# Sliding-window attention ahead of two expert layers: a dilated head's values loaded by a second queue, plain outputs kept in place, copies and denominators divided between VectorE and ScalarE

## The reference

```python
def _attn_ref(q, k, v):                      # each (4, 8, 576, 64): batch, head, position, width
    window, dilation = 32, 4
    scores = scale * np.matmul(q, k.transpose(0, 1, 3, 2))
    rel = pos[:, None] - pos[None, :]
    mask_plain = (rel >= 0) & (rel < window)
    mask_dil = (rel >= 0) & (rel < window * dilation) & (rel % dilation == 0)
    masks = np.stack([mask_plain if h < H // 2 else mask_dil for h in range(H)], axis=0)
    scores = np.where(masks[None, :, :, :], scores, -1000000000.0)
    scores = scores - np.max(scores, axis=-1, keepdims=True)
    attn = np.exp(scores)
    attn = attn / (np.sum(attn, axis=-1, keepdims=True) + 1e-09)
    return np.matmul(attn, v).astype(np.float32)

x = attn_out.transpose(0, 2, 1, 3).reshape(B * S, H * D)   # 2304 token rows of 512
x = _moe_ref(x, ...)       # each row to the best of 8 experts: relu(x @ w1) @ w2, times a gate
return _moe2_ref(x, ...)   # h = x @ w_in; (h * cos(h)) @ w_out
```

## Time and profile before

| | |
|---|---|
| median of 3 runs | 851.77 us (851.12 to 851.94) |
| the profiled execution: its time | 852.95 us |
| its span, first to last instruction | 851.1 us |
| mean granted TensorE clock | 0.996 |
| busy: PE / PEld / DVE / ACT / POOL | 97% / 89% / 72% / 58% / 9% |
| DMA | 93.79 MB, mean 110 GB/s |

### The profile page before, as it was taken

How to read it: one execution, slowest core, us unless ns; L and a number is a source line. 1 busy time by engine, 2 the same in 40 slices (tenths; PEclk the granted TensorE clock), 3 DMA queues, 4 the chain that set the end, 5 groups by cost and what they waited for, 6 DMA issues and landing times.

```text
span 851.1 us, 15552 instructions
## 1 busy us (share of the span) xinstructions
PE 824.1 (97%) x5046; PEld 755.6 (89%) x5046; DVE 610.3 (72%) x1187; ACT 490.4 (58%) x948; POOL 75.5 (9%) x129
## 2 busy tenths in 40 slices
PE   7999999989999999999999999999999999999994
PEld 6877877789999999999989999989999998999993
DVE  6888887885655655555587777798777788777762
ACT  3557767644554554444466666676666676666652
POOL 3122112150100000000000000011000003000002
PEclk9999999999999999999999999999999999999998
DMA  6497886355535434433431221223121214122001
GB/s 149 96 232 177 193 208 183 82 161 161 185 125 162 149 118 131 149 125 123 149 101 59 66 73 52 75 87 112 51 75 50 75 49 149 59 66 68 8 1 74
DMA packets 114913, 93.79 MB, mean 110 GB/s; under 512 B 65816, under 2 KB 94488, under 8 KB 114848
## 3 DMA queue, kind: packets, MB, share of 16 engines
q1 hardware_dynamic: 109920, 78.81, 32.1%
q0 software_dynamic: 4928, 14.16, 5.1%
HBM read 83.51 MB, written 9.44 MB: 109 GB/s over the span
## 4 chain that ended last, share of the span: by engine, by line
PE 86%; DVE 4%; SPq 3%; issue 3%; ACT 2%; DMA 1%; POOL 0%; DVEq 0%; POOLq 0%; ACTq 0%
PE bank L765 25%; PE bank L763 25%; PE bank L764 25%; PE bank L625 2%; PE bank L604 2%; PE bank L588 1%; SPq L378 1%; PE bank L613 1%; SPq L357 1%; DMA xtok<-x_rows 1%; PE bank L805 1%; DVE shifted L1277 1%; DVE row_max L1274 1%; PE bank L706 1%; ACT probs L947 1%
## 5 line engine op out<-in xcount | busy, mean ns | idle before, releaser
L765 PE MATMUL bank<-yh,up_h 128*128 128x384 f32 x384 | 129.6, 338 | 0.0
L763 PE MATMUL bank<-yh,up_l 128*128 128x384 f32 x384 | 129.6, 337 | 0.0
L764 PE MATMUL bank<-yl,up_h 128*128 128x384 f32 x384 | 129.1, 336 | 0.0
L765 PE MATMUL bank<-dn_h,hid 128*128 128x512 f32 x288 | 114.0, 396 | 0.0
L764 PE MATMUL bank<-dn_l,hid 128*128 128x512 f32 x288 | 113.8, 395 | 0.0
L763 PE MATMUL bank<-dn_h,hid 128*128 128x512 f32 x288 | 112.5, 391 | 0.8 <-DVE hid L1604 0.7
L1142 ACT ACTIVATE work<-bank 128x384 f32<-128x384 f32 x96 | 47.2, 491 | 79.6 <-PE bank L765 78.8
L1350 DVE TENSOR_TENSOR dn_l<-dn_raw,dn_h 128x512 fp32r<-128x512 f32 (+1 forms) x79 | 71.8, 909 | 28.1 <-ACT dn_h L998 27.9
L1086 ACT ACTIVATE hid<-bank 128x352 fp32r<-128x352 f32 x64 | 29.8, 465 | 106.4 <-PE bank L765 104.0
L1154 ACT ACTIVATE work<-work 128x384 f32<-128x384 f32 x96 | 50.5, 526 | 64.0 <-DVE work L1599 64.0
L1594 DVE TENSOR_SCALAR work<-work 128x384 f32<-128x384 f32 x96 | 34.7, 362 | 70.6 <-ACT work L1142 70.2
(11 more groups left out here) (213 smaller groups left out, 1727.7 us busy)
## 6 DMA issues: line engine op xcount, KB each, us to landing
up_raw<-in_moe_w_dram SPq DMA_DIRECT2D x32, 512.0 KB, 4.4
dn_raw<-in_moe_w_dram SPq DMA_DIRECT2D x32, 512.0 KB, 3.6
up_raw<-in_moe_w_in_dram SPq DMA_DIRECT2D x24, 512.0 KB, 3.4
dn_raw<-in_moe_w_out_dram SPq DMA_DIRECT2D x24, 512.0 KB, 3.5
qn<-in_q_dram SPq DMA_DIRECT2D x32, 144.0 KB, 2.8
kn<-in_k_dram SPq DMA_DIRECT2D x32, 144.0 KB, 3.3
xtok<-x_rows SPq DMA_DIRECT2D x4, 1152.0 KB, 7.6
x_rows<-osb POOLq DMA_DIRECT2D x8, 288.0 KB, 3.5
```

Source lines behind the costliest of these rows:

```text
L763: mm(o, w[1], x[0], start=first, stop=False, skip_group_check=True)
L764: mm(o, w[0], x[1], start=False, stop=False, skip_group_check=True)
L765: return mm(o, w[0], x[0], start=False, stop=last, skip_group_check=True)
```

## The change

The line numbers in the diff are left out; names are as above.

- **Values of dilated heads.** SyncE loads those of the pair's first head only (four DMAs). GpSimd loads the second head's into the same buffer (`load_second_head`), behind its store of the plain pair two before, counted by a new semaphore `head1_v_in`, for which TensorE waits beside `v_in`.
- **Outputs of plain heads.** The multiply writes them into `xtok` itself, and GpSimd stores them to `x_rows` from there (`plain_stored`, awaited only ahead of the gather). The read-back brings the right half of the columns only, those of the dilated heads.
- **Keys.** VectorE copies the second half of one head (1) only; ScalarE copies that of head 0, a third instruction behind its two, with a semaphore `k_head` for which a pair's first scores wait as well.
- **Denominators.** ScalarE makes them (Copy with bias 1e-9), in each step ahead of the exponential and, where there are any, behind the query copies. VectorE waits for them ahead of the reciprocal.
- **Expert weights.** In the last batch SyncE waits for the second head's last values before it issues the four weight loads.

```diff
...
-    QK_IN, PLAIN_IN, DIL_IN = 16 * 4, 16 * 2 * 3, 16 * 2 * 4
-    STORES = 16 * 5
+    QK_IN, PLAIN_IN, DIL_IN = 16 * 4, 16 * 2 * 3, 16 * 4
+    STORES = 16 * 4
...
-        osb = [sb2(f"osb{i}", [QT, NT, 2, D]) for i in range(2)]
+        osb = [sb2(f"osb{i}", [QT, NT, 2 * D]) for i in range(2)]
...
-        def half_out(copy, p, half, first=False):
-
-            for h in range(2):
+        def half_out(copy, p, half, first=False, heads=(0, 1), signal=None):
+
+            for h in heads:
...
-            last.then_inc(tr_out[half], 1)
+            last.then_inc(signal or tr_out[half], 1)
...
-                        for t, j0, j1, r, i0 in V_PARTS:
+                        for t, j0, j1, r, i0 in V_PARTS if h < 1 else ():
                             sp.dma_start(vw[slot][j0:j1, t:t + 4:3, h, 0:D], vr[r, i0:i0 + j1 - j0]).then_inc(v_in[slot], 16)
...
-                sp.dma_start(xtok[:, bass.ds(last * NT, NT), :],
-                             x_rows[bass.ds(last * S, S), :].rearrange("(t p) c -> p t c", p=QT)).then_inc(x_in, 16)
+                sp.dma_start(xtok[:, bass.ds(last * NT, NT), DM // 2:],
+                             x_rows[bass.ds(last * S, S), DM // 2:].rearrange("(t p) c -> p t c", p=QT)).then_inc(x_in, 16)
...
                         with sp.If(b > B - 2):
+                            sp.wait_ge(head1_v_in[1], B * DIL_IN)
                             load_expert(0, 0, 0, 2)
...
+            def load_second_head(b, p):
+
+                pool.wait_ge(pv_done, b * STEPS + 3 * p + 3)
+                pool.sem_inc(carrier, 1)
+                vr = v[bass.ds(b, 1), 2 * p + 1].rearrange("o (i a r) d -> r i (o a) d", a=2, r=2)
+                for t, j0, j1, r, i0 in V_PARTS:
+                    pool.dma_start(vw[p % 2][j0:j1, t:t + 4:3, 1, 0:D], vr[r, i0:i0 + j1 - j0]).then_inc(head1_v_in[p % 2], 16)
+
...
-                        pool.dma_start(xb.rearrange("(t p) c -> p t c", p=QT), o).then_inc(stored[slot], 16)
+                        pool.dma_start(xb.rearrange("(t p) c -> p t c", p=QT),
+                                       xtok[:, bass.ds(b * NT, NT), 2 * p * D:2 * (p + 1) * D]).then_inc(plain_stored, 16)
+                        load_second_head(b, p + PAIRS // 2)
...
+            pool.wait_ge(plain_stored, B * PAIRS // 2 * 16)
             pool.wait_ge(ids_ready, 1)
...
                         pe.wait_ge(tr_out[half], b * 2 * PAIRS + 2 * p + 3)
+                    pe.wait_ge(k_head, b * PAIRS + p + 1)
...
+                    if p >= PAIRS // 2:
+                        pe.wait_ge(head1_v_in[p % 2], (b + 1) * DIL_IN)
...
                 half_out(lambda o, x: A(o, x, ACT.Copy), p, 0, first)
+                act.wait_ge(tr_done, b * 4 * PAIRS + 4 * p + 12)
+                half_out(lambda o, x: A(o, x, ACT.Copy), p, 1, first, (0,), k_head)
+
+            def denominators(b, s):
+
+                act.wait_ge(pv_done, b * STEPS + (s + 7))
+                act.wait_ge(inv_done, b * STEPS + (s + 3))
+                s %= STEPS
+                A(denom[:, s % 2, :], bank[6 + s % 2][:QT, 0:4 * VN].rearrange("p (a c) -> p a c", a=4)[:, :, D],
+                  ACT.Copy, bias=1e-9).then_inc(denom_done, 1)
...
                         next_pair(b, s, q_out)
+                    if s >= 2:
+                        denominators(b, s - 2)
+                    else:
+                        before_this(act, b, lambda: denominators(b, s - 2))
                     exps(b, s)
...
-                half_out(cp, p, 1, first)
+                half_out(cp, p, 1, first, (1,))
...
+                if p < PAIRS // 2:
+                    rows = xtok[:, bass.ds(b * NT + 2 * u, 2), 2 * p * D:2 * (p + 1) * D]
+                else:
+                    rows = osb[p % 2][:, 2 * u:2 * u + 2, :]
...
-                dve.wait_ge(pv_done, G(7))
-                ts(denom[:, s % 2, :], o[:, :, D], 1e-9, None, ALU.add).then_inc(denom_done, 1)
                 dve.wait_ge(denom_done, G(3))
                 V.reciprocal(inv[:, s % 2, :], denom[:, s % 2, :]).then_inc(inv_done, 1)
...
```

More of the change, by code:

```diff
@@ L199, in fused_kernel @@
         v_in = [sem(f"v_in{i}") for i in range(2)]
+        head1_v_in = [sem(f"head1_v_in{i}") for i in range(2)]
         tr_done = sem_from("tr_done", 8)
         tr_out = [sem_from(f"tr_out{i}", 1) for i in range(2)]
+        k_head = sem("k_head")
         init_v = sem("init_v")
@@ L210, in fused_kernel @@
         denom_done = sem_from("denom_done", 2)
-        inv_done = sem_from("inv_done", 2)
+        inv_done = sem_from("inv_done", 4)
         norm_done = sem_from("norm_done", 4)
         stored = [sem(f"stored{i}") for i in range(2)]
+        plain_stored = sem("plain_stored")
         x_in = sem("x_in")
@@ L521, in _ @@
                     pool.wait_ge(norm_done, b * STEPS + 3 * p + 7)
-                    o = osb[slot][:].rearrange("p t h c -> p t (h c)")
+                    o = osb[slot]
                     xb = x_rows[bass.ds(b * S, S), 2 * p * D:2 * p * D + 2 * D]
                     if p < PAIRS // 2:
-                        pool.dma_start(xb.rearrange("(t p) c -> p t c", p=QT), o).then_inc(stored[slot], 16)
+                        pool.dma_start(xb.rearrange("(t p) c -> p t c", p=QT),
+                                       xtok[:, bass.ds(b * NT, NT), 2 * p * D:2 * (p + 1) * D]).then_inc(plain_stored, 16)
+                        load_second_head(b, p + PAIRS // 2)
                     else:
@@ L988, in _ @@
             probsT_out(B, -1)
+            denominators(B, -2)
+            denominators(B, -1)
             def weights_hi(w, which, raw, hi, i, J, per, slots_free, parts=1, part=0):
@@ L1286, in normalise @@
                 o = bank[6 + s % 2][:QT, 0:4 * VN].rearrange("p (a c) -> p a c", a=4)
-                if u == 0:
-                    if p >= PAIRS // 2:
-                        dve.wait_ge(stored[p % 2], b * STORES + 16)
-                    else:
+                if p < PAIRS // 2:
+                    rows = xtok[:, bass.ds(b * NT + 2 * u, 2), 2 * p * D:2 * (p + 1) * D]
+                else:
+                    rows = osb[p % 2][:, 2 * u:2 * u + 2, :]
+                    if u == 0:
                         def slot_stored():
@@ L1295, in normalise @@
                         before_this(dve, b, slot_stored)
-                dve.wait_ge(pv_done, G(7))
-                ts(denom[:, s % 2, :], o[:, :, D], 1e-9, None, ALU.add).then_inc(denom_done, 1)
                 dve.wait_ge(denom_done, G(3))
                 V.reciprocal(inv[:, s % 2, :], denom[:, s % 2, :]).then_inc(inv_done, 1)
-                dve.wait_ge(inv_done, G(3))
-                tt(osb[p % 2][:, 2 * u:2 * u + 2, :, :].rearrange("p t h c -> p (t h) c"), o[:, :, 0:D],
-                   inv[:, s % 2, :].unsqueeze(2).broadcast_to([QT, 4, D]), ALU.mult).then_inc(norm_done, 1)
+                dve.wait_ge(inv_done, G(5))
+                tt(rows.rearrange("p t (h c) -> p t h c", h=2), o[:, :, 0:D].rearrange("p (t h) c -> p t h c", t=2),
+                   inv[:, s % 2, :].rearrange("p (t h) -> p t h", t=2).unsqueeze(3).broadcast_to([QT, 2, 2, D]), ALU.mult).then_inc(norm_done, 1)
             def over_e(x):
```

## The result

| | before | after |
|---|---|---|
| median of 11 runs each | 852.5 us (851.12 to 855.02) | 847.46 us (846.04 to 849.97) |
| span of the profiled execution | 851.1 us | 845.6 us |
| time less span, wherever both are on record | 1.83 to 1.97 us | 1.49 to 1.60 us |
| ratio | | 0.9934 (0.9922 to 0.9947) |

The ratio on the 851.77 us of the forecast gives 846.1 us: 5.6 us less (4.5 to 6.6), where 3.2 were forecast. Two later measurements of the changed kernel, on other chips, gave 0.9947 (0.9930 to 0.9963) and 0.9923 (0.9898 to 0.9948).

The account below looks back on a forecast made before the run. One latency chain per pair, from scores to exponential and transpose, held back by VectorE's key copies, was taken to set the pace. Start 1.00 and 13 pairs 2.16 gave 3.16 us off 851.77: 848.6 us, range 847.2 to 851.4.

Parts of the forecast that it names:

- The pair's pace, 7.73: Attention, per pair of heads: 7.73 us in place of 7.83, the row maximum waiting for scores alone, if ScalarE keeps up.
- The walk: ScalarE's queue, step by step through a pair: denominators' waits cost nothing; third key copy ends at 81.98, wanted at 82.09.
- Values on two queues: Dilated heads' value loads: SyncE's saved issues bring nothing; GpSimd's loads stay hidden.
- The read-back: Token rows at batch boundaries: 576 KB in place of 1152 land in 5 us, before first use; 0.86 us come back.
- Rival 2: Read-back still late because pieces, not bytes, set its time: the 0.86 us stay, 849.5 us; chance 0.08.
- GpSimd in time with 2.0 us to spare: GpSimd's four value loads: landed some 5.8 us after the multiply, first used 7.83 us after, so hidden.
- ScalarE's slots: Time added on ScalarE: 0.37 us per third key copy, 0.10 per denominator, hidden in the pair, narrowly behind square sums.
- rival 1: ScalarE's slots as long as durations (denominator 0.32, copy 0.41): 1.85 us lost in five pairs, 850.5 us; chance 0.18.
- Rival 3: A pair's first scores wait for ScalarE's third key copy: 0.4 us more per pair, 853.8 us, slower; chance 0.09.
- The address instruction: VectorE, ahead of the multiply into token rows in half the steps: between nothing and 0.1 us, taken as nothing, covered.
- Expert weights: SyncE, last batch: weight loads wait for values until about 134.6, wanted at 144.15; no cost, up to 1 us if stores compete.
- The start, 1.00: First batch, three places where VectorE alone holds it: 0.12, 0.46 and 0.42 us, together 1.00, bounds 0.5 and 1.4.

Follow-up runs that it names:

- both copies shared: Kernel before with denominators and third key copy on ScalarE, values and outputs as before: ratio 1.0005 (0.9985 to 1.0026).
- the run with the filled gap: Changed kernel with the next pair's query transposes and copies one step earlier, where TensorE waits for the third step's exponential: 848.22 us, 0.9933.
- copies undone: Changed kernel with key copies and denominators back on VectorE, split values and direct rows kept: 850.40 us, 0.9990.
- four small additions: Kernel before plus one each: needless copy, semaphore instruction between waits, third key copy's wait, denominator's wait: 853.73, 853.56, 852.98, 851.65 us.

## Why the prediction was right or wrong, point by point

**The bound and the mechanism: right.** The pace was set by the chain from scores to exponential, and VectorE's second key copy held it up. The row maximum now starts 0.04 us after the scores, and TensorE's gap shrank from 0.63 to 0.52 us: the 0.10 of the forecast. The runs with one part agree: with denominators alone VectorE keeps both key copies, and the pair stays at 7.70, 0.12 more than with the third key copy alone.

**The pair's pace, 7.73: wrong by 0.15, the term that made most of the miss.** The step that failed is "In a pair TensorE's weight loads run without a gap except once". There are two gaps. The walk followed the one of 0.63 us, to the exponential and the transposes, and not the one of 0.15 us behind them (83.96 to 84.11), in which TensorE waits for the copy of the previous step's probabilities that stands behind the exponential on ScalarE (ends at 84.06). It was taken as TensorE's own work, which nothing could shorten. In the changed kernel it is gone: from transposes to product 0.38 in place of 0.51 us, 0.13 per pair and 1.7 us over 13. The earlier trace rows had the start of the product, but the trace's rows of its loads and of the copy are not among those of the prediction. Nor did they show that the 0.65 us in front of the copy could shrink, and why it does is not known. But a path that ends with a wait should be followed until the next wait on the same engine is explained as well.

**Values on two queues, "TensorE never waits for values in this trace, so SyncE's saved issues bring nothing": wrong.** It was true of a pair of 7.83 us. At 7.58 the queue of before is too slow in one pair of the first batch, where keys and values come late in the runs with both copies shared, with the third key copy alone and with one queue. I took the new pace from one step of the prediction and the queue's slack from a trace at the old pace. What was short in that pair was issue time: eight loads in 6.00 us on SyncE alone, and four in 2.55 us on GpSimd beside SyncE's four now.

**The read-back: right in what it gave, wrong in what it was worth.** It lands in 4.6 us (estimated 5), and the 0.86 us are gone. Its worth is larger, since at the new pace the whole read-back would be later still: the direct rows undone cost 2.3 us by the medians and 3.0 in the 13 pairs of the profiles, against 0.86 in the sum. In two other runs it came so late that TensorE stood idle for 1.4 and 1.5 us; its clock then fell to 0.51, and a further 1.6 and 1.5 us were lost. Rival 2 is out.

**GpSimd in time with 2.0 us to spare: wrong in the margin.** Four issues take 2.55 us (0.64 each), as forecast. The changed kernel's first profile has no wait for values. But its second has two and its third one, and the prediction had named values among the releasers as a sign of being wrong. The longest, of the second:

```profile
94.73 0.90 PE L643 MATMUL bank<-vw,probsT 128*96 128x72 f32 x8 [0.55 <-DMA vw<-in_v_dram]
```

GpSimd's four loads were issued there from 87.33 to 89.94. The last of them, 64 KB, was issued at 89.21 and landed 5.5 us later, at 94.69. In the other two waits it is the same load, landing at 33.57 and, in the third profile, at 63.89, each 5.1 to 5.2 us after its issue. I had put 2.5, the median. A deadline has to be held against the slow landings.

**ScalarE's slots: right, rival 1 is out.** A denominator took 0.15 to 0.17 us, and the exponential starts 0.07 us behind it (60.52, 60.59); I had taken 0.10.

**Rival 3: not in the changed kernel.** In no pair behind the start does TensorE wait for the third key copy. It is next in line, though: the run with the filled gap shows it at 0.25 us.

**The address instruction: its price was at the upper bound, its cover held.** 0.11 us where 0.1 was the most, hidden, as forecast. Without the cover, with the copies undone, it cost 0.8 us, what the read-back gave.

**Expert weights: no cost that can be told.** SyncE's new wait is long, but hidden. In the first profile it ends 3.5 us after it began, when the last values land (us in total, times, longest):

```profile
SPq L398 <- DMA vw<-in_v_dram: 3.5, 1, 3.5
```

The first weight load is still issued at 127.87, 1.5 us ahead of the last row maximum. From that to the first expert matmul are 45.1 and 45.6 us in two executions before, 45.8, 45.6 and 45.9 in three after: some tenths more at most.

**The start, 1.00: right in size.** With first scores of 1.92 us the sixth row maximum stands at 26.16 before, 25.41 and 25.46 after; with 1.03 us at 23.84 in the second run of the kernel before and 22.84 with both copies shared. 0.7 to 1.0 us. Of the 2.02 us between the two first profiles the rest is luck: TensorE's clock was at its lower level up to 14.2 us in one and from 8.9 to 12.3 us in the other.

**The sum.** Start 0.7 to 1.0. Thirteen pairs: 102.65 and 102.55 before, 98.65, 99.39 and 98.88 after, so 102.60 - 98.97 = 3.6 in place of 2.16. The end: 135.55 - 128.81 = 6.74 before, 129.39 - 122.79 = 6.60 after, 0.14. That is 4.4 to 4.8 us of the span. Another 0.3 is outside it, for which the prediction had nothing: it carried the 1.85 us by which time and span differ before over to the changed kernel, where they differ by 1.49 to 1.60. Why, no trace shows. Together 4.8 to 5.1 us, inside the 4.5 to 6.6 of the timing. Whether there is more I can't say: from the first expert matmul to the end, where nothing is changed, the three profiles of the changed kernel take 670.4, 668.5 and 670.1 us.

**The range** was too narrow below: its low end had nothing for a second wait behind the first (1.7 us), and nothing for the time outside the span (0.3).

## What to carry to other kernels

A change that speeds up a loop shortens every deadline in it; work out the slack of queues and buffers at the new pace, not from the trace at the old one, and expect two parts that are each worth nothing alone to be worth something together. Where an engine waits on a chain, follow it past the first wait to the next one on the same engine. Judge a part of a change by undoing it in the finished kernel as well as by adding it alone: here alone gave 0 and undone gave 2 to 4 us.

## What the runs showed of the hardware that I had not expected

- At the start TensorE's granted clock is on record as 1.00 without a break only from 11.6 to 15.0 us on in most of the kept executions and from near 6 in three of them, and the same four matmuls of the first scores take 1.92 us in the profiled kernel before and 1.03 in its second profile; the start varies by some 2 us with it. The granted clock of a view says 1.00 also where the trace has no record yet, so the lengths of like matmuls have to be looked at.
- In two executions with shared copies a read-back that came late left TensorE idle for 1.4 and 1.5 us, and then its granted clock fell to 0.51 for 3.4 us. The fall cost 1.6 and 1.5 us, as much as the wait itself.
- ScalarE starts one and the same copy 0.54 or 0.65 us behind one and the same exponential, steadily by the place in the program, and with each of four small additions it stayed at 0.65 or 0.66 in 15 third steps, as in the kernel before.
- VectorE's multiply started 0.32 us behind the reciprocal into `xtok`, where a register instruction for the address stands ahead of it, and 0.21 into `osb`, where none does.
- Values loads of 24 to 64 KB landed in 2.1 to 5.5 us within one stretch of 12 us (84 to 96 us in the second profile of the changed kernel).
- The time outside the first and last instruction is not the same for all variants: 1.83 to 1.97 us before, 1.49 to 1.60 as changed, 2.07 to 2.18 with the changed kernel's values on one queue.
